# Attention fused with an MLP: scores from one wide operand, values head by head

## The chip, the cores and the metric

The kernel runs on one core of one Trainium2 chip. The metric is device time in microseconds: three runs of the kernel before gave 1208.76, 1208.96 and 1210.8, median 1208.96. The profiled execution took 1208.68 us. A time is that of the whole program, from launch to the last stored row.

## What is computed

Chunked attention over 4 batches, 8 heads, 768 tokens and a head width of 64, then a gated MLP, then a product of two projections:

```python
# chunks of 32 queries; keys: 8 memory keys, 16 to the left, the chunk, 8 to the right
scores = scale * np.matmul(q_c, k_full.transpose(0, 1, 3, 2))
a = np.exp(scores - np.max(scores, axis=-1, keepdims=True))
a = a / (np.sum(a, axis=-1, keepdims=True) + 1e-09)
out[:, :, c_start:c_end] = np.matmul(a, v_full)
...
h = x @ w_in                                   # 3072 x 512 @ 512 x 2048
g = np.maximum(h, 0.0) + alpha * np.minimum(h, 0.0)
y = g @ w_out                                  # 3072 x 2048 @ 2048 x 512
...
return (y @ w_a) * (y @ w_b) @ w_out2          # widths 1536 and 512
```

## The kernel before, in words

**Precision.** All large products are made of float32r matmuls on operands split into a high part (`_hi`) and what is left (`_lo`): hi·hi + hi·lo + lo·hi, three matmuls (`three`, L612 to L616). ScalarE (ACT) makes the high parts by copying, and GpSimd (POOL) or VectorE (DVE) subtracts to get the low ones. For the scores it is done otherwise: a unit's query and key columns lie twice in the 128 partitions, and GpSimd overwrites the lower 64 query rows with their low part (L548). One matmul of 128 rows with the high keys (L632) then adds (q_hi + q_lo)·k_hi, and a second with the low keys (L633) adds the rest into the same columns.

**Units and tiles.** A unit `u` is one head of 384 tokens in 4 blocks of 96 queries, with 128 keys a block; there are 64 units, 8 to a tile of 384 tokens, 8 tiles. The attention of tile t+1 is worked in between the MLP of tile t. Units 0 to 7 are done ahead in plain float32 (`score_early`, `mix_early`), the 56 others inside `tile`. After tile 7 a last stage does the two projections and their product by a seven-product scheme (`product`, L620 to L622) and `project` (L856 to L858); no line of it is touched.

**Order on TensorE (PE).** It is written out by hand in `tile` (L736 to L763), in pairs of heads. A pair has four `up` (12 matmuls of 384 columns into `h_ps`) and four `down` (12 matmuls into the four `acc` banks) in turn, and behind them: at s = 0 the transposes of the even head (`transpose_probs`, L666) and the scores of the odd head; at s = 4 the transposes of the odd head; at s = 5 the scores of the next even head; at s = 6 both halves of `mix` (L685 to L699). `mix` takes two heads at once: weights are v of one block for both heads (128 columns), moving are the transposed probabilities of both heads (192 columns), and of the 128 x 192 result the two diagonal quarters are used. One half goes to the bank `o_ps`, the other to `pt_ps`, the bank of the transposes. The scores of the four blocks lie side by side in one bank, `s_ps`.

**The other engines.** Each has its own hand-written order with the same semaphores. DVE (L1253 to L1287): `bend` turns an up's bank into `g_raw` by two instructions (L1233, L1238), `split_pt` makes the low part of the transposed probabilities (L1214), `softmax_max` adds the mask to the scores and reduces the maximum in one instruction a block (L1187), `normalise` multiplies by the inverse sums (L1203), `lo_g` makes the low part of g (L1243), `split_x` that of x (L1223, four instructions of 64x192 for a pair). ACT: `split_pt` (L939), `hi_g` (L959), `exps` (L930), `hi_unit` (high parts of a later unit's q, k and v, L893 and L902), `split_x` (L948, four instructions for a pair). POOL: low parts of v, q, k (L537, L548, L553) and, in tile 0, of the MLP's weights (L563). `k_lo` has one buffer, `kq_hi` two. SP's queue issues the loads of units (L385) and weights.

**Who waits for whom.** `down(j)` waits for `g_lo`, `up(j)` for `g_raw` of the up before (the bank must be free), `score(u)` for `k_lo` and for the reduction of the scores before, the transposes for `prob` and for the bank `pt_ps`, `mix` for `pt_lo` and `v_lo`. The first up of a tile waits for `x_lo` of the heads of its columns.

Of the kernel before, what the change touches and what calls it, by code (L numbers as in the profile page):

```python
# [5 lines left out]
F32 = mybir.dt.float32  # L6
# [5 lines left out]
P = 128  # L12
# [44 lines left out]
HALF = TOK // 2  # L57

# [7 lines left out]
def attention_mlp_kernel(nc, units, alpha, w1, w_ab, w_out, y_dram, out):  # L66
    ctx = ExitStack()
    with ctx:
# [27 lines left out]
        v_lo = at("v_lo", AT + 22528, [P, 2, BLOCKS, P], F32R)  # L96
# [57 lines left out]
        h_ps, s_ps, pt_ps, o_ps = bank[4:8]  # L154
        x_ps, y_ps, z_ps, r_ps = (s_ps, pt_ps), (o_ps, h_ps), (bank[0], bank[1]), (bank[2], bank[3])
# [25 lines left out]
        scores = sem("scores")  # L181
        neg_done = sem("neg_done")
# [74 lines left out]
        def half_bank(g, half, early):  # L257

            if early:
                return acc[2 * (g % 2) + half]  # L260
            return pt_ps if half else o_ps
# [260 lines left out]
        def _(pool):  # L522
# [10 lines left out]
            def lo_v(u, c):  # L533

                e, pair = c % 2, (c // 2) % 2
                pool.wait_ge(v_hi_done, pv_count(u))
                nc.gpsimd.tensor_tensor(v_lo[:, pair, 2 * e:2 * e + 2, :],  # L537
                                        raw(u, c % 2)[:, V0:].rearrange("p (i d) -> p i d", i=2),
                                        v_hi[:, pair, 2 * e:2 * e + 2, :].bitcast(F32),
                                        ALU.subtract).then_inc(v_lo_done, 1)  # L540

            def lo_kq(u, c):
# [5 lines left out]
                nc.gpsimd.tensor_tensor(kq_hi[low, b, Q0:], src[low, Q0:V0], kq_hi[low, b, Q0:].bitcast(F32),  # L548
# [4 lines left out]
                nc.gpsimd.tensor_tensor(k_lo[:, :], src[:, 0:Q0], kq_hi[:, b, 0:Q0].bitcast(F32),  # L553
# [57 lines left out]
        def _(pe):  # L611
# [12 lines left out]
            def score(u, b):  # L624
# [29 lines left out]
            def transpose_probs(u, even):  # L654

                pe.wait_ge(prob_done, u + 1)
                if not isinstance(u, int) or u > PV_FIRST:
                    pe.wait_ge(pt_lo_done, pv_count(u, 1))
                elif u:
                    pe.wait_ge(pt_copied, u)  # L660
                if even and (not isinstance(u, int) or u >= HEADS):

                    pe.wait_ge(x_lo_done, u)
# [5 lines left out]
            def mix_early(g, half):  # L669
# [7 lines left out]
                dst = half_bank(g, half, True)  # L677
# [7 lines left out]
            def mix(g, half, pair):  # L685

                pe.wait_ge(pt_lo_done, pv_count(g * 2, -1))
                pe.wait_ge(v_lo_done, pv_count(g * 2, -1))  # L690
                if half == 0:
                    pe.wait_ge(x_lo_done, g * 2)
                dst = half_bank(g, half, False)
                for i in range(2):
                    blk = 2 * half + i
                    last = three(dst[:, i * 2 * QB:(i + 1) * 2 * QB], v_hi[:, pair, blk, :], v_lo[:, pair, blk, :],
                                 pt_hi[:, blk].rearrange("p e q -> p (e q)"),
                                 pt_lo[:, blk].rearrange("p e q -> p (e q)"), True, True)
# [37 lines left out]
            def tile(t, attention):  # L736
# [3 lines left out]
                for p in range(PAIRS):  # L740
                    g = (t + 1) * PAIRS + p
# [806 lines left out]
```

## Time and profile before

| | |
|---|---|
| median of three runs | 1208.96 us |
| the profiled execution | 1208.68 us |
| its span, first to last instruction | 1206.9 us |
| PE busy (matmuls) | 1197.3 us, 99% |
| DVE busy | 722.7 us, 60% |
| ACT busy | 568.8 us, 47% |
| POOL busy | 257.0 us, 21% |
| PE's granted clock, mean | 1.000 of full speed |

The span falls into a prologue (the early units, up to about 42 us), tiles 0 to 7, and the last stage from about 668 us on. A busy PE means only that some matmul was in flight: the records overlap, and the pace has to be read from the distance between the starts of two matmuls. PEld is the loading of weights, which overlaps PE. In the rows below, a group gives busy time and the mean length of one instruction in ns, then the idle time ahead of them and what ended it. A timeline gives start and length in us.

### The profile page before, as it was taken

To read this page: it belongs to the slowest core of one execution; us is meant where nothing else is said; L and a number is where in the kernel's file an instruction comes from. 1 tells how busy PE (TensorE), PEld (TensorE's weight loads), DVE (VectorE), ACT (ScalarE), POOL (GpSimd) and SP (SyncE) were. 2 spreads that over 40 slices of the span, in tenths; PEclk is the share of its full clock that TensorE was granted. 3 is DMA by queue.
4 is the path that set the end of the run, shared out by engine and by line. 5 is a ranking of instruction groups with operands and counts; after the bars stand their busy time and mean duration, and the time that the engine had idled before them with its cause. 6 is when DMAs were issued, how large, how long until landed. Compare 5 with 4: busy or idle time off the path is not lost.

```text
span 1206.9 us, 19092 instructions
## 1 busy us (share of the span) xinstructions
PE 1197.3 (99%) x6611; PEld 1093.2 (91%) x6611; DVE 722.7 (60%) x1772; ACT 568.8 (47%) x1405; POOL 257.0 (21%) x234
## 2 busy tenths in 40 slices
PE   8999999999999999999999999999999999999999
PEld 6899999999999999999999888888888888888887
DVE  6677666666666666666655576744465654566421
ACT  7766454545454545454323454543444443444322
POOL 4885333323333333333035000000000000000000
PEclk9999999999999999999999999999999999999999
DMA  8452222213112222130101501121102121111000
GB/s 301 126 170 71 93 71 71 73 42 100 43 57 87 70 72 73 44 98 28 70 28 36 201 35 70 36 100 66 44 35 71 49 91 62 44 40 66 1 35 35
DMA packets 27843, 87.66 MB, mean 73 GB/s; under 512 B 2752, under 2 KB 7232, under 8 KB 25472
## 3 DMA queue, kind: packets, MB, share of 16 engines
q1 hardware_dynamic: 26576, 85.12, 20.7%
q10 hardware_dynamic: 1200, 1.70, 0.4%
q8 instruction: 36, 0.59, 0.2%
q14 instruction: 31, 0.25, 0.1%
HBM read 74.23 MB, written 12.58 MB: 72 GB/s over the span
## 4 chain that ended last, share of the span: by engine, by line
PE 96%; DVE 2%; POOL 1%; issue 0%; ACT 0%; POOLq 0%; DVEq 0%
PE bank L614 16%; PE bank L616 15%; PE bank L615 15%; PE bank L622 9%; PE bank L620 9%; PE bank L621 9%; PE bank L858 5%; PE bank L857 5%; PE bank L856 5%; PE bank L666 2%; PE bank L633 2%; PE bank L632 1%; POOL w_first L563 0%; DVE y_stage L1187 0%; DVE prob L1203 0%
## 5 line engine op out<-in xcount | busy, mean ns | idle before, releaser
L621 PE MATMUL bank<-yc,ws 128*128 128x512 f32 x504 | 196.1, 389 | 0.0
L622 PE MATMUL bank<-yc,ws 128*128 128x512 f32 x504 | 196.1, 389 | 0.0
L620 PE MATMUL bank<-yc,ws 128*128 128x512 f32 x504 | 196.1, 389 | 0.0
L1233 DVE TENSOR_SCALAR g_neg<-bank,al 128x384 f32<-128x384 f32 x128 | 79.1, 618 | 178.3 <-PE bank L616 178.3
L959 ACT ACTIVATE g_hi<-g_raw 128x384 fp32r<-128x384 f32 x128 | 67.3, 525 | 119.9 <-DVE g_raw L1238 119.9
L930 ACT ACTIVATE prob<-prob,neg_max 96x128 f32<-96x128 f32 x220 | 85.6, 391 | 73.6 <-DVE neg_max L1187 73.6
L621 PEld LDWEIGHTS bank<-yc,ws 128*128 128x128 f32 x504 | 94.6, 188 | 19.7
L622 PEld LDWEIGHTS bank<-yc,ws 128*128 128x128 f32 x504 | 94.6, 188 | 19.6
L620 PEld LDWEIGHTS bank<-yc,ws 128*128 128x128 f32 x504 | 94.6, 188 | 19.5
L1432 DVE TENSOR_TENSOR p_split<-p_all,p_split 128x512 fp32r<-128x512 f32 x72 | 49.5, 691 | 93.6 <-ACT p_split L1102 93.4
L1102 ACT ACTIVATE p_split<-p_all 128x512 fp32r<-128x512 f32 x72 | 45.2, 631 | 110.3 <-PE bank L858 100.8
L553 POOL TENSOR_TENSOR k_lo<-u_raw,kq_hi 128x512 fp32r<-128x512 f32 x53 | 68.5, 1293 | 116.6 <-PE bank L633 116.0
L614 PE MATMUL bank<-x_hi,w_first 128*128 (+1 forms) x256 | 86.9, 340 | 2.4 <-POOL w_first L563 1.6
L614 PE MATMUL bank<-g_hi,w_later 128*128 128x384 f32 x256 | 88.0, 344 | 0.5 <-DVE g_lo L1243 0.5
L614 PE MATMUL bank<-g_hi,w_first 128*128 128x384 f32 x256 | 88.0, 344 | 0.2 <-DVE g_lo L1243 0.2
L537 POOL TENSOR_TENSOR v_lo<-u_raw,v_hi 128x256 fp32r<-128x256 f32 x53 | 44.5, 839 | 198.7 <-ACT v_hi L902 198.7
L614 PE MATMUL bank<-x_hi,w_later 128*128 (+1 forms) x256 | 86.4, 338 | 0.0
L616 PE MATMUL bank<-g_hi,w_first 128*128 128x384 f32 x256 | 85.9, 335 | 0.0
L616 PE MATMUL bank<-g_hi,w_later 128*128 128x384 f32 x256 | 85.9, 335 | 0.0
L615 PE MATMUL bank<-g_lo,w_first 128*128 128x384 f32 x256 | 85.8, 335 | 0.0
L615 PE MATMUL bank<-g_lo,w_later 128*128 128x384 f32 x256 | 85.8, 335 | 0.0
L615 PE MATMUL bank<-x_lo,w_first 128*128 (+1 forms) x256 | 85.7, 335 | 0.0
(152 smaller groups left out, 2991.1 us busy)
## 6 DMA issues: line engine op xcount, KB each, us to landing
u_raw<-units SPq DMA_DIRECT2D x53, 576.0 KB, 3.7
wr<-w_ab SPq DMA_DIRECT2D x18, 1024.0 KB, 4.8
out<-o_stage SPq DMA_DIRECT2D x23, 256.0 KB, 2.0
u_early<-units SPq DMA_DIRECT2D x10, 576.0 KB, 9.3
y_dram<-y_stage SPq DMA_DIRECT2D x6, 768.0 KB, 4.6
y_stage<-w SPq DMA_DIRECT2D x16, 256.0 KB, 2.9
wr<-y_dram SPq DMA_DIRECT2D x8, 512.0 KB, 4.2
w_raw<-w SPq DMA_DIRECT2D x12, 256.0 KB, 3.0
```

What stands on the lines that cost most here:

```text
L553: nc.gpsimd.tensor_tensor(k_lo[:, :], src[:, 0:Q0], kq_hi[:, b, 0:Q0].bitcast(F32), ALU.subtract).then_inc(k_lo_done, 1)
L614: nc.tensor.matmul(out_ap, w_hi, m_hi, start=first, stop=False)
L615: nc.tensor.matmul(out_ap, w_hi, m_lo, start=False, stop=False)
L616: return nc.tensor.matmul(out_ap, w_lo, m_hi, start=False, stop=last)
L620: nc.tensor.matmul(out_ap, w_hi, m_hi, start=first, stop=False, skip_group_check=True)
L621: nc.tensor.matmul(out_ap, w_hi, m_lo, start=False, stop=False, skip_group_check=True)
L622: return nc.tensor.matmul(out_ap, w_lo, m_hi, start=False, stop=True, skip_group_check=True)
L856: nc.tensor.matmul(r_ps[u % 2][:, :], hi, w[:, 0], start=g == order[0] and c == 0, stop=False)
L857: nc.tensor.matmul(r_ps[u % 2][:, :], hi, w[:, 1], start=False, stop=False)
L930: last = nc.scalar.activation(dst[:, i, :], src[:, i, :], ACT.Exp, bias=neg_max[:, b, i:i + 1], scale=-1.0, accum_out=row_sum[:, b, i, 0:1])
L959: nc.scalar.activation(g_hi[:, j % 2], g_raw[:, :], ACT.Copy).then_inc(g_hi_done, 1)
L1233: nc.vector.tensor_scalar(g_neg[:, :], h_ps[:, 0:TOK], 0.0, al[:, j:j + 1], ALU.min, ALU.mult)\
```

## The change

Four things, all in the attention of units 8 to 63.

1. **Scores.** The high keys of the two buffers and the low keys lie in one tensor, `kq` = high 0, low, high 1, so that one access pattern with two parts reaches the high and the low keys of a block (`k_parts`; for buffer 0 high comes first, for buffer 1 low). One matmul of 2 x 128 moving columns takes the place of L632 and L633, and writes the two products side by side instead of adding them up. They need two banks: blocks 0 and 1 in `s_ps`, blocks 2 and 3 in `o_ps`.
2. **The sum on DVE.** `softmax_max_parts` first adds the low products of two blocks to the mask, in one instruction a bank (two of 96x256), waits for that on its own semaphore `low_added`, and then reduces block by block as before, with the sum in place of the mask.
3. **Values head by head.** `mix(u, c)` does one head: per block a weight of 64 columns (v of one head) and 96 moving columns, three matmuls a block, twelve a head, into partitions 0 to 63 of `pt_ps`. v lies by head in four slots, and is packed so on the host for units 8 to 63. ACT and DVE take x from the bank by one instruction of 64x384 each a head (in place of two of 64x192 a head).
4. **The order** becomes one of single heads: up, transposes(u), scores(u+1), down, up, mix(u), down; DVE and ACT follow. The transposes wait for `x_lo` of the head before, since `mix` uses their bank; `mix` no longer waits for `x_lo`.

The core of the diff:

```diff
-        kq_hi = at("kq_hi", AT + 9216, [P, 2, V0], F32R)
-        k_lo = at("k_lo", AT + 16384, [P, Q0], F32R)
-        v_hi = at("v_hi", AT + 18432, [P, 2, BLOCKS, P], F32R)
+        kq = at("kq", AT + 9216, [P, 2 * V0 + Q0], F32R)
+        kq_hi = [kq[:, 0:V0], kq[:, V0 + Q0:]]
+        k_lo = kq[:, V0:V0 + Q0]
+        k_parts = [kq[:, 0:2 * V0].rearrange("p (s c) -> p s c", s=2),
+                   kq[:, V0:V0 + 2 * Q0].rearrange("p (s c) -> p s c", s=2)]
+        v_hi = at("v_hi", AT + 18432, [P, V_SLOTS, BLOCKS * HEAD_DIM], F32R)
...
+        s_banks = (s_ps, o_ps)
...
+        def score_parts(k, b):
+            both = s_banks[k][0:QB, :].rearrange("p (i s k) -> p i s k", i=2, s=2)
+            return both[:, :, b, :], both[:, :, 1 - b, :]
...
             def score(u, b):
...
                 for i in range(BLOCKS):
-                    q = kq_hi[:, b, Q0 + i * QB:Q0 + (i + 1) * QB]
-                    at = slice(i * KEYS, (i + 1) * KEYS)
-                    nc.tensor.matmul(s_ps[0:QB, at], q, kq_hi[:, b, at], start=True, stop=False)
-                    last = nc.tensor.matmul(s_ps[0:QB, at], q, k_lo[:, at], start=False, stop=True)
+                    q = kq_hi[b][:, Q0 + i * QB:Q0 + (i + 1) * QB]
+                    dst = s_banks[i // 2][0:QB, (i % 2) * 2 * KEYS:(i % 2 + 1) * 2 * KEYS]
+                    last = nc.tensor.matmul(dst.rearrange("p (s k) -> p s k", s=2), q,
+                                            k_parts[b][:, :, i * KEYS:(i + 1) * KEYS], start=True, stop=True)
...
-            def transpose_probs(u, even):
+            def transpose_probs(u):
                 pe.wait_ge(prob_done, u + 1)
                 if not isinstance(u, int) or u > PV_FIRST:
-                    pe.wait_ge(pt_lo_done, pv_count(u, 1))
+                    pe.wait_ge(x_lo_done, u)
...
+            def mix(u, c):
+                pe.wait_ge(pt_lo_done, pv_count(u))
+                pe.wait_ge(v_lo_done, pv_count(u))
+                e, slot_v = c % 2, c % V_SLOTS
+                for i in range(BLOCKS):
+                    d = slice(i * HEAD_DIM, (i + 1) * HEAD_DIM)
+                    last = three(pt_ps[0:HEAD_DIM, i * QB:(i + 1) * QB], v_hi[:, slot_v, d], v_lo[:, slot_v, d],
+                                 pt_hi[:, i, e, :], pt_lo[:, i, e, :], True, True)
+                last.then_inc(mixed, 1)
...
+                for c in range(HEADS):
+                    u = (t + 1) * HEADS + c
+                    up(t, 2 * c, x_at, first)
+                    if attention:
...
+                        transpose_probs(u)
+                        if attention == 2 or c < HEADS - 1:
+                            score(u + 1, (c + 1) % 2)
+                    if c:
+                        down(t, 2 * c - 1, first)
...
+                    up(t, 2 * c + 1, x_at, first)
+                    if attention:
+                        mix(u, c)
+                    down(t, 2 * c, first)
...
+            def softmax_max_parts(u, b, half):
+                dve.wait_ge(scores, u + 1)
+                dve.wait_ge(transposed, u)
+                for k in range(2):
+                    last = nc.vector.tensor_tensor(prob[:, 2 * k:2 * k + 2, :], score_parts(k, b)[1],
+                                                   mask[:, half + 2 * k:half + 2 * k + 2, :], ALU.add)
+                last.then_inc(low_added, 1)
+                dve.wait_ge(low_added, u - HEADS)
+                for i in range(BLOCKS):
+                    last = nc.vector.tensor_tensor_reduce(
+                        out=prob[:, i, :], in0=score_parts(i // 2, b)[0][:, i % 2, :], in1=prob[:, i, :], scale=-SCALE,
+                        scalar=FAR, op0=ALU.add, op1=ALU.min, accum_out=neg_max[:, b, i:i + 1])
+                last.then_inc(neg_done, 1)
...
# DVE's tile, one head
+                    bend(t, 2 * c, first)
+                    if attention:
+                        split_pt(u, c % 2)
...
+                    if more:
+                        softmax_max_parts(u + 1, (c + 1) % 2, half if c < HEADS - 1 else half_after)
+                    if not (first and c == 0):
+                        lo_g(t, 2 * c)
+                    if c == 0 and not first:
+                        empty_y(t - 1)
+                    bend(t, 2 * c + 1, first)
+                    if more:
+                        normalise(u + 1, (c + 1) % 2)
+                    if attention:
+                        split_x(u, c, x_at)
+                    lo_g(t, 2 * c + 1)
```

`split_x` on DVE and ACT now works on `pt_ps[0:HEAD_DIM, 0:TOK]` and writes the 64 rows of its head in x.

## Rows read from the trace of the kernel before

**Rows 1.** The page: busy time of each engine, and the chain that ended last by engine.

```profile
PE 1197.3 (99%) x6611; PEld 1093.2 (91%) x6611; DVE 722.7 (60%) x1772; ACT 568.8 (47%) x1405; POOL 257.0 (21%) x234
...
PE 96%; DVE 2%; POOL 1%; issue 0%; ACT 0%; POOLq 0%; DVEq 0%
```

**Rows 2.** The chain in order of time: start us, us, what; two transposes of the same kind.

```profile
114.79 0.33 PE bank L666 x4
...
538.43 0.33 PE bank L666 x4
```

**Rows 3.** Timeline of PE: start us, us, line, operation; one up, transposes, scores, the next down.

```profile
253.76 0.33 PE L614 MATMUL bank<-x_hi,w_later 128*128 x1
...
255.84 0.49 PE L666 MATMUL bank<-ident,prob 96*128 96x96 f32 x4
...
256.24 0.25 PE L633 MATMUL bank<-k_lo,kq_hi 128*96 128x128 f32 x1
...
256.83 0.39 PE L614 MATMUL bank<-g_hi,w_later 128*128 128x384 f32 x1
257.06 0.33 PE L615 MATMUL bank<-g_lo,w_later 128*128 128x384 f32 x1
```

**Rows 4.** Timeline of PE: the twelve value matmuls of a pair of heads, and what follows.

```profile
250.33 0.25 PE L614 MATMUL bank<-pt_hi,v_hi 128*128 128x192 f32 x1
...
251.64 0.36 PE L614 MATMUL bank<-g_hi,w_later 128*128 128x384 f32 x1
251.84 0.34 PE L615 MATMUL bank<-g_lo,w_later 128*128 128x384 f32 x1
```

**Rows 5.** Groups by line and form: busy us, mean ns | idle before us, and releaser.

```profile
L1233 DVE TENSOR_SCALAR g_neg<-bank,al 128x384 f32<-128x384 f32 x128 | 79.1, 618 | 178.3 <-PE bank L616 178.3
...
L632 PE MATMUL bank<-kq_hi 128*96 128x128 f32 x220 | 41.9, 249 | 0.0
L1223 DVE TENSOR_TENSOR x_lo<-bank,x_hi 64x192 fp32r<-64x192 f32 x128 | 45.3, 354 | 2.5 <-ACT x_hi L948 0.7
...
L614 PE MATMUL bank<-pt_hi,v_hi 128*128 128x192 f32 x112 | 29.9, 267 | 0.0
L1214 DVE TENSOR_TENSOR pt_lo<-bank,pt_hi 128x384 fp32r<-128x384 f32 x56 | 30.7, 548 | 0.0
```

**Rows 6.** Timeline of PE in the last stage: matmuls of 512 columns.

```profile
901.35 0.39 PE L621 MATMUL bank<-yc,ws 128*128 128x512 f32 x1
...
903.85 0.39 PE L620 MATMUL bank<-yc,ws 128*128 128x512 f32 x1
```

**Rows 7.** Timeline of PEld: loads of 96 columns, then of 128.

```profile
256.69 0.17 PEld L633 LDWEIGHTS bank<-k_lo,kq_hi 128*96 128x96 f32 x1
256.77 0.19 PEld L614 LDWEIGHTS bank<-g_hi,w_later 128*128 128x128 f32 x1
256.88 0.19 PEld L615 LDWEIGHTS bank<-g_lo,w_later 128*128 128x128 f32 x1
```

**Rows 8.** Busy time of each engine in the steady stretch (42 heads).

```profile
114.80:537.90 423.10, 423.10 (x2770) 421.52 (x2769) 275.31 (x852) 213.53 (x642) 132.68 (x126) 1.00 0.21 70
```

**Rows 9.** One line's instructions: duration in ns, least/median/most.

```profile
L1243 DVE TENSOR_TENSOR g_lo<-g_raw,g_hi x128: 543/550/1636, 34.2 to 662.5; 128x384 fp32r<-128x384 f32 x128
```

**Rows 10.** Timeline of PE, first microseconds: 64-row matmuls, entered and left.

```profile
4.29 0.70 PE L651 MATMUL bank<-u_early 64*96 64x128 f32 x3
...
4.94 0.60 PE L651 MATMUL bank<-u_early 64*96 64x128 f32 x4
5.47 0.39 PE L640 MATMUL bank<-const-bfloat16-1.0 128*128 128x512 bf16 x1
...
6.77 0.54 PE L651 MATMUL bank<-u_early 128*96 128x128 f32 x3 [0.26 <-DVE neg_max L1187]
...
7.26 0.60 PE L651 MATMUL bank<-u_early 128*96 128x128 f32 x4
7.70 0.38 PE L640 MATMUL bank<-const-bfloat16-1.0 128*128 128x512 bf16 x1
```

More of the change, by code:

```diff
@@ L57 @@
 HALF = TOK // 2
+V_SLOTS = 4
 Q0 = BLOCKS * KEYS
@@ L255, in pv_count, with half_bank @@
             return u - (PV_FIRST - 1 + behind)
[L257 to L261, printed above, removed]
+        def half_bank(g, half):
+            return acc[2 * (g % 2) + half]
+        def score_parts(k, b):
+            both = s_banks[k][0:QB, :].rearrange("p (i s k) -> p i s k", i=2, s=2)
+            return both[:, :, b, :], both[:, :, 1 - b, :]
         def stage_of(n):
@@ L676, in mix_early @@
                     pe.wait_ge(early_loaded[0], 16)
-                dst = half_bank(g, half, True)
+                dst = half_bank(g, half)
                 for i in range(2):
@@ L683, in mix_early @@
                 last.then_inc(mixed, 1)
[L685 to L698, printed above, removed]
+            def mix(u, c):
[6 more added lines that the diff above has]
+                                 pt_hi[:, i, e, :], pt_lo[:, i, e, :], True, True)
                 last.then_inc(mixed, 1)
@@ L984, in weights @@
                             hi_w(n)
-                for p in range(PAIRS):
-                    g = (t + 1) * PAIRS + p
-                    more = attention == 2 or p < PAIRS - 1
-                    odd_loads = t * (HEADS // 2) + (p + 1)
-                    split_pt(g * 2, 0)
-                    hi_g(t, 4 * p, first)
-                    weights(4 * p)
-                    if p == 0 and not first:
-                        empty_y(t - 1)
-                    exps(g * 2 + 1, 1, prob, prob)
-                    if more:
-                        hi_unit(g * 2 + 3, 2 * p + 3, odd_loads)
-                    hi_g(t, 4 * p + 1, first)
-                    weights(4 * p + 1)
-                    split_pt(g * 2 + 1, 1)
-                    hi_g(t, 4 * p + 2, first)
-                    weights(4 * p + 2)
-                    if more:
-                        exps(g * 2 + 2, 0, prob, prob)
-                    hi_g(t, 4 * p + 3, first)
-                    split_x(g, 0, p, x_at)
-                    split_x(g, 1, p, x_at)
-                    if attention == 2 or p < PAIRS - 2:
-                        hi_unit(g * 2 + 4, 2 * p + 4, odd_loads)
-                    weights(4 * p + 3)
+                for c in range(HEADS):
+                    u = (t + 1) * HEADS + c
+                    split_pt(u, c % 2)
+                    hi_g(t, 2 * c, first)
+                    weights(2 * c)
+                    if c == 0 and not first:
+                        empty_y(t - 1)
+                    if attention == 2 or c < HEADS - 1:
+                        exps(u + 1, (c + 1) % 2, prob, prob)
+                    if attention == 2 or c < HEADS - 3:
+                        hi_unit(u + 3, c + 3, t * (HEADS // 2) + (c // 2 + 1))
+                    hi_g(t, 2 * c + 1, first)
+                    split_x(u, c, x_at)
+                    weights(2 * c + 1)
             for u in range(HEADS + 1):
```

144 lines of the change are left out of this document (56 added, 88 removed).

## The prediction

> **What bounds the kernel now.** I read the page's busy times and chain first [rows 1]: TensorE (PE) is busy for 99% of the span and holds 96% of the chain that ended last, while VectorE (DVE) is busy for 60% and ScalarE (ACT) for 47%. So a microsecond off PE's stream is a microsecond off the end, as long as nobody else becomes late; work added to DVE costs nothing until PE waits for it. Next the chain in order of time, to get the period [rows 2]: two transposes of the same kind stand at 114.79 and 538.43, and 42 heads lie between, so 423.64 / 42 = 10.087 us a head.
>
> Then PE's timeline inside a period. Twelve matmuls of 384 columns run from 253.76 to 255.84, so one starts every 0.1733 us [rows 3]; a record's own length (0.33) is its latency and says nothing of the pace. The transposes start at 255.84, the scores end before the L614 at 256.83, and the matmul behind that starts at 257.06. Without attention it would have started one step after 255.84, so transposes and scores together cost 257.06 - 255.84 - 0.173 = 1.047 us. Within it, seven score matmuls lie between 256.24 and 256.83: 0.0843 each. By the same reckoning the twelve value matmuls of two heads cost 251.84 - 250.33 - 0.173 = 1.337 us, 0.669 a head, at (251.64 - 250.33) / 12 = 0.109 each [rows 4]. Check: 48 x 0.1733 + 1.047 + 0.669 = 10.03 a head against 10.087 measured; 0.05 us stays unexplained, and I carry it over unchanged.
>
> How often: 220 matmuls of L632 are 55 heads of scores, 112 first value matmuls are 56 heads [rows 5]. Heads 0 to 7 go another way, and the change does not touch it. Nor does it touch the last stage, which begins when the scores are long over.
>
> **The scores.** Eight matmuls a head (96 weight columns, 128 moving) become four with 256 moving columns. Removed: 8 x 0.0843 = 0.674. Price of a 256-column matmul: no row has that width. The neighbours are 384 columns at 0.1733 and 512 columns at (903.85 - 901.35) / 11 = 0.2273 [rows 6]; the line through them gives 0.1733 - 128 x 0.000422 = 0.119. From below it can't be under the 0.0843 of 128 columns, from above not over two of those, 0.169. I take 0.119, since both neighbours are streams of the same data type; four make 0.477. There is a second term. The load of weights ahead of the next big matmul: with 96 columns the loads stand 0.08 apart, the one after the 128-column load is 0.11 behind, though the matmul that runs in front has 128 columns in both cases [rows 7]. So short matmuls go at the pace of their weight loads, and the first wide load after the scores sticks out by some 0.026. Behind a 0.119 matmul it no longer does. Saved: 0.674 - 0.477 + 0.026 = 0.223 a head, x 55 = 12.3 us.
>
> **The values.** Six matmuls a head (128 weight columns, 192 moving) become twelve of 64 and 96. By the same reading the load decides: 0.11 for 128 columns (rows 7, and the 0.109 above), 0.084 for 96, a step of 0.026 for 32 columns, hence 0.058 for 64. The stream's line of rows 3 and 6 gives 0.053 for 96 columns, which is the lower end; the upper end is 0.084, should a narrower load save nothing more. I take 0.058, because the two rows with their loads exposed are this operation and its nearest kin. The first wide load behind them then sticks out by 0.11 - 0.058. Cost: 12 x 0.058 + 0.052 = 0.748 against 0.669: +0.079 a head, x 56 = +4.4 us. Transposes stay four a head.
>
> **DVE.** Each head gains two additions of a bank's low half with the mask, 96x256 from PSUM. Between 354 ns for 192 columns and 548 ns for 384 [rows 5], 256 columns come to about 0.42, so 0.84, plus a wait of DVE on itself, for which no row stands; it is above zero and below a whole addition, and I put it at 0.1. The low part of x becomes one 384-column subtraction (0.548) in place of two of 0.354: -0.16. Together +0.78 a head. In the steady stretch DVE works 275.31 of 423.10 us, so it idles 3.5 us a head [rows 8]; after the change (0.78 more work, 0.15 less period) it idles 2.6. ACT loses one instruction a head (one 384-column copy for two of 192), and has its later unit's high parts (L893, L902) between the exponentials and the g_hi of every head now, not once on each side of a pair's middle; it works 213.53 / 42 = 5.1 of 10.1 us a head, so I cost that at nothing too. POOL and SP's queue keep their counts, sizes and order. All of this lies beside PE and is costed at nothing. Its cover is DVE's idle time, most of which is waiting for the next up (L1233 in rows 5); if that were gone, all 0.78 x 55 = 43 us would show.
>
> **The waits.** DVE works in halves, from one bend (L1233) to the next, in order. Behind the summing and reducing of the scores stands, in its queue, the g_lo that a down needs; in the other half x_lo and a g_lo stand behind the normalising. Today DVE idles 178.3 / 128 = 1.4 us ahead of each bend, waiting for PE's up [rows 5]. The half with the additions gets 0.94 longer and the period of two halves 0.15 shorter, so some 0.4 us of that idle time stays there; the other half loses only the 0.07. And g_lo is not due when the next bend is: PE still has the value matmuls (0.75), or the transposes and scores (0.82), between that up and the down that takes it. So a half may run 1.1 us over before PE waits. The transposes of every head, not of every second one, now wait for x_lo of the head before, as values and transposes share a bank; scores and a down are queued behind them, and they are due at the end of the up, so here only the idle time ahead of the bend (1.3) is in hand, plus the 0.55 of the g_lo that follows x_lo. What could use that up is POOL: a g_lo of 543 ns at best takes up to 1636 [rows 9], and tile 0 has POOL splitting weights all along. One such hit fits, two in one half don't; I add 0.3 us for that tile. Sum: -12.3 + 4.4 + 0.3 = -7.6 us.
>
> **Rivals.**
>
> *The narrow value matmuls drain the array (slower).* A 64-column output may be handled as a tile of its own, with a pause on entering and leaving. The trace has one such pair, in rows instead of columns [rows 10]: from the first of four records to the next L640 it takes 5.47 - 4.94 = 0.53 after 64-row matmuls and 7.70 - 7.26 = 0.44 after 128-row ones, 0.09 more; and three records on entering take 0.70 against 0.54, 0.16 more. That is 0.25 a head, x 56 = +14 us, and 1208.7 - 7.6 + 14 = 1215.1. It decides from 0.14 us a head. Against it: the pair in rows 10 may owe part of its 0.16 to the wait ahead of it, and none of it is a column case. The Trainium skill says under "TensorEngine Tiling (Array Packing)", Key Properties, that changing the tiling mode drains TensorE, which here would happen twice a head; by "PSUM — Partial Sum Buffer", on the zero region of a first matmul, float32r matmuls always name all column groups, and then no change of mode would occur. No row here shows which holds.
>
> *Short matmuls have a floor.* No two float32r matmuls in these rows go at a pace below 0.084 us. If that is a floor and not the width, the twelve cost 11 x 0.084 + 0.11 = 1.034, and 0.286 x 56 = 16 us come on top of my sum: 1217. It decides from 0.07 a matmul. Against it: the step between 96 and 128 columns in rows 7. For it, the Trainium skill's "TensorE: Matmul & The Clock Gate" (Back-to-back issue gap) has about 81 ns for each load and matmul of 128 columns in a long stream, which would make 12 of them 0.97.
>
> *DVE is late.* If waits on g_lo or x_lo of 0.05 to 0.2 us come with each head, 3 to 11 us go: 1204 to 1212, most likely about 1206. For it: rows 9, and DVE goes from 65% to 74% in the stretch. Against it: the 1.1 us that each half may run over.
>
> *The two halves of the wide operand stream no faster than two matmuls* (0.169, the upper bound): the 12.3 us are not saved and the 4.7 are paid: 1213.4.
>
> **The numbers.** The profiled execution took 1208.68 us (span 1206.9 and 1.8 around it), 0.3 below the median of 1208.96. From it: 1208.7 - 7.6 = 1201.1. Forecast 69%, drain 7%, floor 8%, late DVE 12%, no faster wide stream 4%. The forecast's own range: with 0.053 a value matmul and 0.115 a score matmul 3.5 us less, with 0.062 a value matmul 3 us more, 1197.5 to 1204. The range has to reach over late DVE to hold 8 in 10: 1196.5 to 1210. About 0.2%, 2.4 us, is what can be told from no change here. Faster: the forecast and most of late DVE, 0.76. Within it: the rest of late DVE, 0.05. Slower: drain, floor and the wide stream, 0.19.
>
> **What the profile after would show.** Right: a period near 9.94 us; score matmuls 0.12 apart, value matmuls 0.058 apart, no idle time ahead of either; PE at 99%. Drain: a gap ahead of the first value matmul and ahead of the next down. Floor: even steps of 0.084. Late DVE: PE idle ahead of L614 with g_lo or x_lo as releaser, above all in tile 0. The prediction is wrong if the period is above 10.05 us, or if the last stage changes its length.

## The result, and the profile after

| | before | after |
|---|---|---|
| median of the runs taken together | 1208.86 us (1208.74 to 1210.8) | 1195.49 us (1195.14 to 1196.86) |
| span of the profiled execution | 1206.9 us | 1193.6 us |
| period of a head in the steady stretch | 10.087 us | 9.880 us |

The ratio is 0.9888 (0.9871 to 0.9905): 13.4 us less, where I forecast 7.6 less. The sign and the mechanism hold, the size does not, and the time lies 1.0 us under the range (1196.5 to 1210). A second set of runs of the same kernel gave 1195.23 (ratio 0.9882, 0.9866 to 0.9897).

The page of the kernel after, the rows that answer to [rows 1]: PE as full as before, DVE up by 55.7 us.

```profile
PE 1185.7 (99%) x6725; PEld 1080.3 (91%) x6727; DVE 778.4 (65%) x1826; ACT 557.5 (47%) x1349; POOL 279.2 (23%) x234
...
PE 97%; POOL 1%; DVE 1%; DMA 0%; issue 0%; ACT 0%; POOLq 0%; DVEq 0%
```

The chain in order of time (start us, us, what), answering to [rows 2]. One head is 9.88 us from the first two rows on, in tile 0 as in the middle; in [rows 2] one had to average over 42 heads.

```profile
61.73 0.33 PE bank L673 x4
71.61 0.33 PE bank L673 x4
...
506.33 0.33 PE bank L673 x4
516.21 0.33 PE bank L673 x4
```

PE's timeline (start us, us, line, operation): transposes and scores, as in [rows 3], then the value matmuls of a head, as in [rows 4].

```profile
254.25 0.20 PE L623 MATMUL bank<-pt_hi,v_hi 128*64 128x96 f32 x1
...
254.88 0.22 PE L625 MATMUL bank<-pt_hi,v_lo 128*64 128x96 f32 x1
254.94 0.40 PE L623 MATMUL bank<-g_hi,w_later 128*128 128x384 f32 x1
255.18 0.34 PE L624 MATMUL bank<-g_lo,w_later 128*128 128x384 f32 x1
...
259.17 0.49 PE L673 MATMUL bank<-ident,prob 96*128 96x96 f32 x4
259.45 0.68 PE L641 MATMUL bank<-kq 128*96 128x256 f32 x4
259.97 0.34 PE L623 MATMUL bank<-g_hi,w_later 128*128 128x384 f32 x1
260.15 0.33 PE L624 MATMUL bank<-g_lo,w_later 128*128 128x384 f32 x1
```

Read as in the prediction: transposes and scores cost 260.15 - 259.17 - 0.173 = 0.81 us (0.804 as a mean over forty heads; forecast 0.824, before 1.047 by one reading), the values 255.18 - 254.25 - 0.173 = 0.757 (0.751 as a mean; forecast 0.748), at (254.94 - 254.25) / 12 = 0.0575 each. Neither an idle bracket nor a gap stands ahead of the first value matmul or behind the last. And 48 x 0.1733 + 0.804 + 0.751 = 9.87 for a period of 9.88: next to nothing stays unexplained here, where before 0.05 us did.

DVE's groups of the kernel after (busy us, mean ns | idle before us, releaser): the two new additions and the wait for the next up, which [rows 5] have at 178.3.

```profile
L1241 DVE TENSOR_SCALAR g_neg<-bank,al 128x384 f32<-128x384 f32 x128 | 79.1, 618 | 129.2 <-PE bank L625 129.2
```
```profile
L1183 DVE TENSOR_TENSOR prob<-bank,mask 96x256 f32<-96x256 f32 x16 | 5.9, 410 | 0.0
```

The second row is of the window 42 to 115 us. DVE took in 110 additions of 410 ns (45 us), and 49 us of its idle time ahead of the bends went.

**Where the time came from**, by the start of the first transposes of head 8, 10, 16 and 62 (tile 0 is heads 8 to 15), all in us:

| stretch | before | after | change | forecast |
|---|---|---|---|---|
| start to head 8 | 32.55 | 32.97 | +0.42 | 0 |
| heads 8 to 10 | 20.10 | 18.72 | -1.38 | -0.29 |
| heads 10 to 16 | 61.99 | 59.28 | -2.71 | -0.86 + 0.3 |
| heads 16 to 62, each | 10.0867 | 9.8800 | -9.51 | -6.6 |
| rest up to the last stage | 83.91 | 83.80 | -0.11 | -0.07 |
| last stage | 544.37 | 544.37 | 0 | 0 |

The start swings by itself: over the profiled executions below head 8 begins at 32.4 to 33.0 us or at 34.3 to 34.5, and the total moves with it, by up to 2 us. The executions of the kernel before lie in two groups accordingly, 1208.6 to 1209.7 and 1210.4 to 1210.9, and the median of a set can fall into either. The two medians above are both of the early group. In the experiments they are not always, so a difference of medians under 2 us says little there, and sizes are read stage by stage, by this table's method.

Two misses, then: 0.063 us a head in the steady stretch, and tile 0, where heads 8 to 16 gained 4.09 us, 1.65 by the new period and 2.43 beyond it, instead of losing 0.3.

The chain of the kernel before in tile 0 shows the second (start us, us, what). Every second head there, three times in all, it leaves PE:

```profile
59.38 0.18 DVE inv_sum L1198
59.59 1.57 DVE prob L1203
61.16 1.57 DVE g_lo L1243
...
62.77 0.44 PE bank L614
```

A normalising that takes 0.69 us as a median took 1.57, and the g_lo queued behind it as long, and PE's down waited. The chain of the kernel after has no DVE piece between 50 and 112 us, though its DVE is no faster there (g_lo is slower, the normalising a little shorter). DVE's groups in the window 50 to 112, before and then after:

```profile
L1243 DVE TENSOR_TENSOR g_lo<-g_raw,g_hi 128x384 fp32r<-128x384 f32 x13 | 10.5, 811 | 0.4
L1203 DVE TENSOR_TENSOR prob<-prob,inv_sum 96x512 f32<-96x512 f32 x6 | 6.9, 1158 | 0.2
L1238 DVE SCALAR_TENSOR_TENSOR g_raw<-bank,g_neg 128x384 f32<-128x384 f32 x12 | 6.7, 558 | 0.4
```
```profile
L1251 DVE TENSOR_TENSOR g_lo<-g_raw,g_hi 128x384 fp32r<-128x384 f32 x13 | 14.1, 1081 | 0.1
L1204 DVE TENSOR_TENSOR prob<-prob,inv_sum 96x512 f32<-96x512 f32 x6 | 6.4, 1062 | 0.2
```

A second wait of tile 0 stands in heads 8 to 10: PE waits once for a weight that POOL splits into high and low part. PE's timeline of the kernel before, of the kernel after, and of e4 (below; the kernel before with POOL as it was):

```profile
39.70 0.41 PE L614 MATMUL bank<-x_hi,w_first 128*128 128x384 f32 x1 [1.62 <-POOL w_first L563]
39.64 0.41 PE L623 MATMUL bank<-x_hi,w_first 128*128 128x384 f32 x1 [0.39 <-POOL w_first L572]
39.60 0.41 PE L614 MATMUL bank<-x_hi,w_first 128*128 128x384 f32 x1 [1.12 <-POOL w_first L563]
```

Counted from the start of head 8, PE comes to this matmul at 5.52 us in the kernel before and at 6.28 in the kernel after, because head 8's value matmuls now stand ahead of it. The split is there at 6.64 to 6.67 us in some executions and at 7.13 to 7.15 in others, of either kernel: e4 has 6.64, the kernel before 7.15, the kernel after 6.67, e2 (the kernel after without some work of DVE) 7.13. So of the 1.23 us that this wait lost, 0.75 are the order, and 0.48 are chance.

### The profile page after: what moved, and what is told of

Its sections match the earlier page's. It is cut to its first block, busy times and chain, and to the rows that moved or that the text cites. A ratio compares the mean times of both kernels' runs of the same rounds, so it can differ in the third digit from the quotient of the medians.

```text
span 1193.6 us, 19240 instructions
## 1 busy us (share of the span) xinstructions
PE 1185.7 (99%) x6725; PEld 1080.3 (91%) x6727; DVE 778.4 (65%) x1826; ACT 557.5 (47%) x1349; POOL 279.2 (23%) x234
## 4 chain that ended last, share of the span: by engine, by line
PE 97%; POOL 1%; DVE 1%; DMA 0%; issue 0%; ACT 0%; POOLq 0%; DVEq 0%
PE bank L623 16%; PE bank L625 16%; PE bank L624 16%; PE bank L630 10%; PE bank L631 10%; PE bank L629 10%; PE bank L852 5%; PE bank L851 5%; PE bank L853 5%; PE bank L641 2%; PE bank L673 2%; POOL w_first L572 0%; DVE y_stage L1173 0%; DMA u_early<-units 0%; PE bank L660 0%
## 5 line engine op out<-in xcount | busy, mean ns | idle before, releaser
L1251 DVE TENSOR_TENSOR g_lo<-g_raw,g_hi 128x384 fp32r<-128x384 f32 x128 | 95.0, 742 | 10.5 <-ACT g_hi L957 9.5
L931 ACT ACTIVATE pt_hi<-bank 128x384 fp32r<-128x384 f32 x56 | 27.6, 492 | 157.7 <-PE bank L673 157.6
L562 POOL TENSOR_TENSOR kq<-u_raw,kq 128x512 fp32r<-128x512 f32 x53 | 69.3, 1307 | 96.0 <-PE bank L641 95.4
L548 POOL TENSOR_TENSOR v_lo<-u_raw,v_hi 128x256 fp32r<-128x256 f32 x53 | 41.9, 790 | 187.2 <-ACT v_hi L896 187.2
```

The costliest lines, as they stand in the source:

```text
L562: nc.gpsimd.tensor_tensor(k_lo, src[:, 0:Q0], kq_hi[b][:, 0:Q0].bitcast(F32), ALU.subtract).then_inc(k_lo_done, 1)
L1251: nc.vector.tensor_tensor(g_lo[:, j % 2], g_raw[:, :], g_hi[:, j % 2].bitcast(F32), ALU.subtract)\
```

## The experiments

"Period" is heads 16 to 62 by the table's method. "Late steps" are steps from one 384-column matmul to the next, behind a group of attention matmuls, that take longer than 0.1733 us; the first step behind the group is counted with the group. Their figure is the sum of what they take over 0.1733.

**1. The wide operand alone, undone** (after, the same layout, eight matmuls of 128 columns again).

```diff
-    last = nc.tensor.matmul(dst..., q, k_parts[b][:, :, i * KEYS:(i + 1) * KEYS], start=True, stop=True)
+    for s in range(2):
+        last = nc.tensor.matmul(dst[:, s * KEYS:(s + 1) * KEYS], q,
+                                k_parts[b][:, s, i * KEYS:(i + 1) * KEYS], start=True, stop=True)
```

> The changed kernel (1195.5 us), with the one wide score matmul of a block undone alone: two matmuls of 128 columns write the same two places; banks, additions on VectorE, values and order stay. Theory L (short matmuls that are bound by their weight loads cost more than their pace: the first wide load behind them, and a delay of some 29 ns spread over the next six big matmuls): transposes and scores go from 0.80 to 1.047 a head plus the 0.029, 0.276 x 55 = 15 us, 1210.7. Rival R (the reading of the prediction: pace and first wide load are all, and the 0.05 us a head that was left unexplained belongs to the period and not to the scores): 0.223 x 55 = 12.3 us, 1207.8.

Measured: 1210.88 (ratio 1.0004, 0.9994 to 1.0013), period 10.140, +0.260 a head. The median looks like the higher of the two expected times (1210.7), but it is of the late group; four of the ten executions took 1209.0 to 1209.5, some 14 us over the kernel after. The period decides: 0.260 lies between the expected 0.223 and 0.276, nearer the second. So the wide operand is worth more than my 0.223, and without it the rest of the change gains nothing. Of the 0.260, 0.234 is in transposes and scores (1.039 for 0.804, means over some forty heads), and 0.026 is time that no score matmul holds. It shows in PE's timeline of this kernel, behind the scores:

```profile
264.81 0.87 PE L642 MATMUL bank<-kq 128*96 128x128 f32 x8
265.52 0.39 PE L623 MATMUL bank<-g_hi,w_later 128*128 128x384 f32 x1
...
266.26 0.35 PE L624 MATMUL bank<-g_lo,w_later 128*128 128x384 f32 x1
266.45 0.34 PE L625 MATMUL bank<-g_hi,w_later 128*128 128x384 f32 x1
266.63 0.34 PE L623 MATMUL bank<-g_hi,w_later 128*128 128x384 f32 x1
266.81 0.33 PE L624 MATMUL bank<-g_lo,w_later 128*128 128x384 f32 x1
```

The step is 0.1733 in a long run; here it is 0.19 at 266.26 and 0.18 at 266.45 and 266.63. Over thirty such groups of the kernel before, the steps behind the first wide one are 173.7, 174.6, 177.5, 185.0, 175.9 and 181.6 ns, in sum 28 ns over 6 x 173.3 (26 where the transposes stand right ahead of the scores, 31 where they don't); behind transposes alone or the value matmuls of a pair, 11 ns. In the kernel after they are 173.3 from the second step on behind scores, and 4 ns over behind values.

This kernel settles something on tile 0 too: it has the narrow scores and the new order, and its heads 10 to 16 take 60.84 us, six times 10.140. The waits on g_lo went with the order, not with the wide operand.

**2. DVE without the additions** (after; this leaves the low products out of the scores).

```diff
-    last = nc.vector.tensor_tensor(prob[...], score_parts(k, b)[1], mask[...], ALU.add)
-    ...
-        ... in1=prob[:, i, :]
+        ... in1=mask[:, half + i, :]
```

> The changed kernel without VectorE's two additions a head; the product of the low keys is computed and left out of the scores. If the additions are hidden, as the trace after says (no wait of TensorE on VectorE in the steady part): 1195.5 within 0.5. If they delay it somewhere in a way that the waits do not show: 1 to 3 us faster.

Measured: 1196.62 (0.9887, 0.9871 to 0.9904), period 9.880, the same to the nanosecond: the 0.82 us of additions a head cost nothing in the steady stretch. The median is 1.1 us above the kernel after, outside the 0.5 expected. The profiled execution shows where: head 8 began at 34.53 us for 32.97, heads 8 to 10 took 0.46 longer by the later split, and from head 10 on not a stage differs.

**3. How much more would fit** (after, the additions done three times; experiment 11 puts one thing in another place on ACT besides).

```diff
 # e3
-    for k in range(2):
-        last = nc.vector.tensor_tensor(...)
+    for r in range(3):
+        for k in range(2):
+            last = nc.vector.tensor_tensor(...)
 # e11, on top of it
-    hi_unit(u + 3, ...)
     hi_g(t, 2 * c + 1, first)
     split_x(u, c, x_at)
+    hi_unit(u + 3, ...)
```

> The changed kernel with the two additions done three times over, each pair behind a wait for the one before: 1.7 us more of VectorE a head. If a half of VectorE's work may run over the start of its next bend by what TensorE still has ahead of the down (1.2 us idle and 0.75 of value matmuls, 1.95 in all): between 0 and 10 us slower, 1196 to 1205, with small waits on g_lo or x_lo. If the idle time ahead of the bend (1.2) is all the cover there is: 0.5 x 55 = 27 us slower, 1223.

> e3_adds_x3 (the changed kernel with the low-part additions done three times, 1.7 us more on DVE a head, 1215.8) with one thing moved on ACT: the high parts of the unit of three heads ahead (kq and v) come behind x_hi instead of ahead of the second g_hi. Theory from e3's trace (PE waits because additions push back the exponentials, these push back the unit's high parts, g_hi and x_hi, and so x_lo, which the next transposes wait for): x_hi comes 1.0 us earlier against the rest, DVE no longer waits 0.85 to 0.98 us for it, the period falls from 10.20 to 9.88 to 10.0, and the time to 1197 to 1205. Rival (DVE itself is full at three times the additions: its chain of bends and g_lo sets the period): nothing gained, 1215 to 1216.

Measured: e3 1215.81 (1.0042, 1.0028 to 1.0056), period 10.200; it lies between its two expectations, and neither was right. e11 1202.96 (0.9944, 0.9928 to 0.9961), period 10.010, about as expected (1197 to 1205, up to 10.0). ACT's timeline of e3, then DVE's (the bracket is the idle time before and its releaser):

```profile
256.23 0.94 ACT L888 ACTIVATE kq<-u_raw 128x896 fp32r<-128x896 f32 x1
257.07 0.40 ACT L896 ACTIVATE v_hi<-u_raw 128x256 fp32r<-128x256 f32 x1
257.38 0.51 ACT L957 ACTIVATE g_hi<-g_raw 128x384 fp32r<-128x384 f32 x1
257.91 0.48 ACT L937 ACTIVATE x_hi<-bank 64x384 f32 x1
```
```profile
256.76 0.69 DVE L1205 TENSOR_TENSOR prob<-prob,inv_sum 96x512 f32<-96x512 f32 x1
258.43 0.55 DVE L1223 TENSOR_TENSOR x_lo<-bank,x_hi 64x384 fp32r<-64x384 f32 x1 [0.98 <-ACT x_hi L937]
259.01 0.78 DVE L1252 TENSOR_TENSOR g_lo<-g_raw,g_hi 128x384 fp32r<-128x384 f32 x1
```

So with 1.7 us more DVE is not full: it waits 0.98 us for ACT, whose exponentials came late (behind the additions), with 1.3 us of high parts that nobody needs yet queued behind them. With these put last, the x_hi is there when DVE comes, and 0.19 of the 0.32 us a head is won back. What is left, 0.13 a head or 1.04 a tile, stands in one place: the second to eighth head of a steady tile take 9.88 us, the first 10.9. There PE has one wait, in the waits of e11 (us in total, times, longest):

```profile
PE bank L623 <- DVE y_stage L1260: 4.8, 6, 0.8
```

**4, 5, 6. Orders in tile 0.** e4: before, g_lo ahead of the normalising in tile 0. e5: before, POOL's first two weight splits ahead of unit 10's low parts. e6: the same in the kernel after.

```diff
 # e4
+    if first:
+        lo_g(t, 4 * p + 1)
     if attention:
         normalise(g * 2 + 1, 1)
 # e5 and e6, on POOL, for j = 0
+    for n in w_in_tile0(0):
+        lo_w(n)
     lo_unit(HEADS + 2, 2)
```

> The kernel before (1208.9), with one swap on VectorE in tile 0: g_lo of every second up ahead of the normalising, not behind it. Theory L, its part on tile 0 (three pairs there lose 0.5 us each because the down that stands behind only an up and four transposes waits for a g_lo behind a normalising that POOL slows down; in the changed kernel the value matmuls and the scores stand in between and cover it): the three waits go, 1.5 us faster, 1207.4. Rival (POOL's slowing down of VectorE costs this whatever the order): 1208.9.

> The kernel before, with the first two weight splits of tile 0 on POOL (L563, slots 4 and 5) ahead of unit 10's low parts, not behind them. If TensorE's wait of 1.6 us on L563 at 39.7 us is a place in POOL's queue: 1.6 us faster, 1207.3; the changed kernel has 0.75 us of value matmuls there and waits 0.4. If the next load or ACT is late as well: under 0.5 us faster.

> The changed kernel with the same swap on POOL: its wait on the same split is 0.4 us, so 0.4 faster, 1195.1; if the order on POOL was not the cause, no change.

Measured: e4 1209.42 (1.000, 0.9991 to 1.0009), so no gain. Heads 10 to 16 took 62.93 us for 61.99 (and heads 8 to 10 0.48 less, by the earlier split alone). The wait only moved to what had been put last:

```profile
PE bank L666 <- DVE prob L1203: 1.8, 3, 0.6
```

e5 1207.73 (0.999, 0.9981 to 0.9999), against 1207.3 expected. PE's wait of 1.6 us on the split is gone, so that wait was a place in POOL's queue; but PE waits 0.94 us on head 9's transposes for an x_lo instead, and heads 8 to 10 take 19.32 us for 20.10, half of the gain expected there. Another 0.42 came in heads 10 to 16, where one of the three waits on g_lo went. e6 1196.27 (0.9889, 0.9873 to 0.9904): heads 8 to 10 in 18.14 for 18.72, but its time is not told apart from 1195.49; its profiled start came 1.4 us later.

**7, 8. What sets the pace of the value matmuls** (after, with 128 and with 32 weight columns in each of the twelve; e7 takes the next block's columns in as well (block 3 uses block 2's) and so computes other values, e8 leaves half of each head's columns out).

```diff
-    v_hi[:, slot_v, d], v_lo[:, slot_v, d]      # d: 64 columns
+    v_hi[:, slot_v, d], v_lo[:, slot_v, d]      # e7: d of 128 columns, e8: of 32
```

> The changed kernel with 128 weight columns in each value matmul in place of 64 (v of two blocks; the second half of the result is overwritten or left unused, and block 3 uses the columns of block 2), the 96 moving columns unchanged. If the weight load sets the pace: 0.111 instead of 0.058 apart, 12 x 0.053 x 56 = 35 us slower, about 1230. If the stream of 96 columns or a floor sets it: 1195.5.

> The changed kernel with 32 instead of 64 weight columns in each of the 12 value matmuls of a head (this leaves half of each head's value columns out). If the weight load sets their pace, as the 64-column pace of 0.058 us against 0.109 at 128 columns says, the load falls to about 0.03 and the stream of 96 columns, 0.053 by the scale of 0.1733 for 384 with the constant part taken out, sets it: 12 x 0.005 = 0.06 us a head, 3.4 us in all, 1192. If each matmul had a floor above 0.055 us, nothing changes: 1195.5. If the stream of 96 columns could go at 0.040 (96/2.4), 12 x 0.018 = 0.22 us a head, 1183.

Measured, one run each: e7 1230.75, period 10.493 (+0.613 x 56 = 34 us); e8 1188.23, period 9.753 (-0.127 x 56 = -7.1). PE's timelines of e7 and of e8:

```profile
268.82 0.27 PE L625 MATMUL bank<-pt_hi,v_lo 128*128 128x96 f32 x1
268.93 0.28 PE L623 MATMUL bank<-pt_hi,v_hi 128*128 128x96 f32 x1
269.04 0.28 PE L624 MATMUL bank<-pt_lo,v_hi 128*128 128x96 f32 x1
```
```profile
251.40 0.21 PE L625 MATMUL bank<-pt_hi,v_lo 128*32 128x96 f32 x1
251.45 0.21 PE L623 MATMUL bank<-pt_hi,v_hi 128*32 128x96 f32 x1
...
251.59 0.21 PE L623 MATMUL bank<-pt_hi,v_hi 128*32 128x96 f32 x1
```

With the same 96 moving columns, 128 weight columns go at 0.11 us, 64 at 0.0575, 32 at (251.59 - 251.40) / 4 = 0.0475 in these lines and at 0.046 as a mean over forty heads. From 128 to 64 the pace halves: the load sets it. From 64 to 32 it no longer does; something near 0.046 takes over, either the stream of 96 columns or a floor. These runs don't tell which, but a floor of 0.084 is out. Of e7's +0.613, 0.022 are late steps behind the value matmuls (0.026 for 0.004), so these steps are not peculiar to scores. All three figures of my expectation for e8 missed: 0.053 was too high for the stream, 0.040 too low.

**9, 10. Why tile 0 gained** (before, with the even head's scores directly behind the odd head's transposes; and before, with POOL writing zeros in place of the subtractions of tile 0's weights).

```diff
 # e9, on PE
     elif s == 4:
         transpose_probs(g * 2 + 1, False)
-    elif s == 5 and (attention == 2 or p < PAIRS - 1):
-        score(g * 2 + 2, 0)
+        if attention == 2 or p < PAIRS - 1:
+            score(g * 2 + 2, 0)
 # e10, on POOL
-    nc.gpsimd.tensor_tensor(slot(n)[:, 1], w_stage(n), slot(n)[:, 0]..., ALU.subtract)
+    nc.gpsimd.memset(slot(n)[:, 1]..., 0.0)
```

> The kernel before, with one thing moved on TensorE: the scores of the next even head come directly behind the odd head's transposes (as all scores do in the changed kernel), ahead of the down group that waited for its g_lo behind the slow normalise in tile 0, instead of behind it. It gives DVE 0.70 us more before that down group. Theory (the waits of tile 0 in the kernel before came from the order, a g_lo behind a normalise with too little PE work to cover it): the three waits of 0.5 us go, heads 10 to 16 take 60.5 us instead of 61.99, and one transition from transposes to large matmuls less per pair gives 0.01 to 0.04 us a head in the steady part: 1206 to 1207. Rival (POOL and DVE slow each other down, and any order waits for them): the waits move to another line, as they did in e4_before_glo_first, heads 10 to 16 stay at 61.9 or more, and only the transition's part is seen, 1208 to 1209.

> The kernel before, with the sixteen pairs of weight low parts that POOL subtracts in tile 0 written as zeros by POOL instead (this leaves the low halves of those weights out of the computation; every other instruction and wait stays). If the slow normalise (1.57 us for a 96x512 product that takes 0.69 us in its fastest form) and the slow g_lo come from POOL's subtractions beside DVE's, both fall to their fast forms, the waits of tile 0 go, heads 10 to 16 take 60.5 us and heads 8 to 10 under 19.3 us: 1206.0 to 1207.3. If the order alone makes the waits, DVE's durations stay and so does 1208.9.

Measured, beside a median of 1210.49 for the kernel before: e9 1206.19 (0.9974, 0.9963 to 0.9985), e10 1206.17 (0.997, 0.9958 to 0.9983). The 1210.49 is of the late group and the other two of the early one (the early executions before took 1208.8 to 1209.3), so the gain is not 4.3 us but 2.7 in each by the stages. Both came as the theory had them, each by one half of the cause. In e10 heads 10 to 16 take 60.52 us, six times the steady 10.087, and DVE's groups of the same window read:

```profile
L1239 DVE SCALAR_TENSOR_TENSOR g_raw<-bank,g_neg 128x384 f32<-128x384 f32 x12 | 6.7, 558 | 0.4
L1244 DVE TENSOR_TENSOR g_lo<-g_raw,g_hi 128x384 fp32r<-128x384 f32 x12 | 6.6, 551 | 0.4
L1204 DVE TENSOR_TENSOR prob<-prob,inv_sum 96x512 f32<-96x512 f32 x6 | 4.1, 687 | 0.2
```

So it is POOL's subtractions that stretch the normalising (1158 to 687) and g_lo (811 to 551), while g_raw, which reads PSUM, stays at 558 either way. The Trainium skill has this under "SBUF — State Buffer", Who interferes with whom: a DVE instruction with two SBUF inputs contends with a GpSimd instruction that reads SBUF, and not with one that only writes it. The traces agree in the first part: two SBUF inputs were slowed, and g_raw, with one, was not. Of the second they show little: three g_lo of e10 had a memset beside them and took 547 to 548 ns, and no normalising had one.

In e9 nothing on DVE got faster. Its timeline in tile 0, then PE's:

```profile
59.78 1.57 DVE L1203 TENSOR_TENSOR prob<-prob,inv_sum 96x512 f32<-96x512 f32 x1
61.27 1.64 DVE L1243 TENSOR_TENSOR g_lo<-g_raw,g_hi 128x384 fp32r<-128x384 f32 x1
```
```profile
62.05 0.34 PE L616 MATMUL bank<-x_hi,w_first 128*128 128x384 f32 x1
62.22 0.49 PE L666 MATMUL bank<-ident,prob 96*128 96x96 f32 x4
62.50 0.28 PE L632 MATMUL bank<-kq_hi 128*96 128x128 f32 x1
```

The g_lo ends at about 62.9, as late against its up as before, but PE has 0.70 us of scores to do in the meantime, and heads 10 to 16 take 60.38 us, six times 10.063. The period fell too, by 0.023 us a head: an odd head's transposes and scores standing together are cheaper by 0.047 a pair than with a down between them, of which 0.031 is in the pieces themselves and 0.016 in the late steps behind them.

## Why the prediction was wrong, step by step

All figures here are us a head, means over the groups between 150 and 540 us (19 of each form before, about 40 after):

| part | before | after | change | forecast |
|---|---|---|---|---|
| transposes and scores | 1.054 (1.038 joined, 1.069 apart) | 0.804 | -0.249 | -0.223 |
| values | 0.671 | 0.751 | +0.080 | +0.079 |
| late steps behind either | 0.039 | 0.004 | -0.035 | 0 |
| sum with 48 x 0.1733 | 10.084 | 9.879 | -0.205 | -0.144 |
| period measured | 10.087 | 9.880 | -0.207 | |

**The scores** (forecast -0.223). Where transposes and scores stand side by side they went from 1.038 to 0.804: -0.234. The line through 384 and 512 columns was the right one of the bounds, for a 256-column matmul goes at 0.116, not 0.119; the 0.011 that I missed is in the wide load behind the scores, which stuck out by 0.050 before (0.006 after), not by 0.026. Right, and 0.011 too small.

**The values** (forecast +0.079): +0.080. The pace of 0.058 read off the weight loads was right, and experiments 7 and 8 show that the load is its cause.

**"0.05 us stays unexplained, and I carry it over unchanged": this step failed**, and it is the miss of the steady stretch. The 0.05 belonged to what the change removes. One part is the odd head's transposes and scores standing apart: I had measured only the joined group and counted it for both heads, and apart they cost 0.031 a pair more, 0.015 a head. The other is the late steps, 0.039 a head before and 0.004 after: most of them stand behind the eight narrow score matmuls and come back when experiment 1 narrows them again, the rest behind transposes that stood alone and behind the values. Together 0.050, in place of nothing, and with the 0.011 of the scores it makes 0.061 of the 0.063 that I missed a head. (e9's gain of 0.023 is the 0.015 and 0.008 of the late steps.) My 0.05 itself was a little small, as the one group that I read gave 1.047 where the mean is 1.038. Over the 54 heads from 8 to 62 the 0.063 is 3.4 of the 5.7 us that I was off.

**Tile 0: "I add 0.3 us for that tile": this failed too**, by 2.7 us. I asked only whether the change would add waits, and didn't look for those that stood there already. I had the slow g_lo in [rows 9] and saw POOL as a danger for the kernel after; it was a cost of the kernel before. The joined order of the change takes it away, as e9 does in the kernel before: DVE is as late, and PE has the scores in between. That is 1.47 us of heads 10 to 16. The other 0.96, of heads 8 to 10, goes with PE's first wait on a POOL weight split, 1.6 us before and 0.4 after. It is the same mechanism once more, 0.75 us of value matmuls put ahead of a waiting matmul, as read from the traces above; no run isolates it. And 0.48 of it is luck: the split came early in the profiled execution of the kernel after and late in that of the kernel before. (The two make 1.23, the stretch gained 0.96; where the other 0.27 went stays open.) Against that luck stands the start, 0.42 us later in the kernel after. e5 and e10 take the wait down through POOL alone (heads 8 to 10 shorter by 0.78 and 1.23), so it is POOL that PE waits for there.

**DVE's additions at nothing** was right (experiment 2), but DVE's work was mis-sized. From 110.97 to 525.93 us, 42 heads of the kernel after, DVE is busy for 319.4 us, 7.605 a head in place of 6.555 [rows 8]: +1.05, not +0.78. A g_lo takes 729 ns there for 550, and a normalising 969 for 820: in the new order more of them run beside POOL's subtractions for the units (past tile 0, 45 of 100 g_lo against 6 of 96, and 45 of 47 normalisings against 23), and a g_lo beside one takes 923 ns on the mean, alone 551. This was hidden as well: PE waits for neither. That **"a half may run 1.1 us over before PE waits"** left ACT out: by e3 and e11 the limit lies first in the order of ACT's queue. At the change's own size it isn't reached. That ACT's later unit costs nothing was therefore right only because the additions left room.

**The rivals.** Drain: no gap ahead of the value matmuls or behind them, and their cost of 0.751 leaves no room for 0.25. The Trainium skill's rule that a change of tiling mode drains TensorE ("TensorEngine Tiling (Array Packing)", Key Properties) does not show for 64-column outputs here. What the Trainium skill says in "PSUM — Partial Sum Buffer", on the zero region, that float32r matmuls are forced to name all column groups, fits with there being no change of mode; that last step is my inference. Floor: paces of 0.0575 and 0.046 are both below 0.084. They are also below the 81 ns of the Trainium skill's "TensorE: Matmul & The Clock Gate", Back-to-back issue gap, for a load and a matmul, which is for 128 columns. By the LDWEIGHTS section of the same page of the Trainium skill a load takes its number of columns divided by 1.2, in ns, which makes 107, 53 and 27 ns as estimates for 128, 64 and 32 columns. The traces have paces of 110, 57.5 and 46, so the rule holds nearly where the load sets the pace, and not at 32. Late DVE: in the kernel after PE never waits on g_lo, and once, 0.8 us, on an x_lo of the prologue, as in the kernel before. The wide operand no faster: it fell with the pace of 0.116, far from 0.169.

**The range** ended 1.0 us above the result. Its lower end was made of paces alone (and those add up to 4.0 us less by my own terms, 12 x 0.005 - 0.005 a head for the values and 4 x 0.004 for the scores, not 3.5); it held nothing for the 0.05 being part of the change (2.8 us), nor for waits of the kernel before that the new order might remove. Either of the two misses alone, 3.4 or 2.7 us, would have left the time within the range.

## What to carry to other kernels

A remainder between the sum of your parts and the measured period belongs to somebody: before carrying it over, compare the steps behind each kind of group with the steady step, and measure every form in which a group stands, as a mean over many and not from one reading that is good to 0.01 us. When a change reorders PE's queue, list the waits of the kernel before that stand beside the reordered pieces, because a piece of PE work put ahead of a waiting matmul can pay for itself, as it did in tile 0. For narrow matmuls read the pace from the weight load as long as it is the slower part (here down to 64 columns, no longer at 32). One operand that covers two products saved a load here, and the additions that it needs elsewhere were free because DVE had idle time; how many more would be depended on the order of ACT's queue too. And when whole executions fall into two groups, compare stages and not medians.

## What the runs showed of the hardware that I had not expected

- Behind eight score matmuls that go at the pace of their loads, the 384-column matmuls don't return at once to 173.3 ns: seven steps on they are still at 181.6, 28 ns lost in all. Behind the 256-column score matmuls nothing of it is seen. Behind e7's twelve value matmuls (128 weight, 96 moving columns, 0.11 us apart) it is 26 ns, behind the twelve of the kernel before (128 and 192 columns, 0.109 apart) only 11. So being bound by the loads is not all of it; the cause stays open.
- Transposes and scores with a down between them cost 0.047 us a pair more than side by side.
- A moving operand in two parts of 128 columns goes at 0.116 us, no more than the line through contiguous 384 and 512 columns gives (0.119): no price of the break between the parts is seen. A contiguous one of 256 columns was not run beside it.
- With 96 moving float32r columns and 32 weight columns the pace was 0.046 us (e8, one run); no narrower weights were tried.
- An engine's work can slow another's by where it stands: DVE's g_lo went from 550 to 729 ns on the mean in the steady stretch with no edit to it, by running beside POOL more often.
